# Router scores of the second mixture out of the first mixture's weights: one kernel, before and after

## The chip, the cores and the metric

The kernel runs on one core of a Trainium2 chip. The metric is device time in microseconds of one execution; lower is better. Its engines are TensorE (PE in the profile, its weight loads PEld), VectorE (DVE), ScalarE (ACT), GpSimd (POOL) and SyncE (SP), each with its own queue of instructions; they wait for each other by semaphores only.

## The reference

```python
x = attn(x, weight)            # 4 x 3584 tokens of D = 192; per head softmax(weight) over 7 taps, causal convolution
# first mixture: x is passed through where x @ w_skip <= 0
xc = x[x @ w_skip > 0]
e = argmax(xc @ w_gate); g = softmax(xc @ w_gate)[e]
out = xc + g * (relu(xc @ w1[e]) @ w2[e])         # w1: 192 x 1024, w2: 1024 x 192, 8 experts
# second mixture, all 14336 tokens
e = argmax(x @ w_gate2); g = softmax(x @ w_gate2)[e]
o = sigmoid(x @ w_output_gate2)[e]
out = g * o * (relu(x @ w1_2[e]) @ w2_2[e])
```
Everything is float32. The input of the second mixture's router is the output of the first mixture.

## The kernel before

**Routing.** The tokens are taken in 16 groups (B = 4 batches, GPB = 4) of 7 windows of 128 tokens. For a group SyncE loads the windows (load_windows), TensorE convolves them with Toeplitz matrices (conv, L963, and the halo, L971), ScalarE copies the result into `rows` (rows_out, L527), TensorE transposes the rows (L1026, L1027), ScalarE copies them to x1A and x1B (L545, L546), and TensorE multiplies by routerA and routerB, which hold w_skip, the first mixture's gates and the second's two sets of gates (L1037). The scores are transposed (scores_of, L1006), VectorE chooses the expert, TensorE counts ranks (ranks_of, L993, L995), VectorE works out a slot for each token, and GpSimd scatters each window's rows, with gate and token number behind the 192 values, to a bucket in HBM: seven indirect DMAs a group (L440). Scores, ranks and slots of a group are made in the pass of the next group. `rows` has a buffer for each q of 0 to 3, so rows of group n wait for the scatter of group n-4. A token that skips the first mixture goes straight to a bucket of the second.

**Tiles.** Buckets are read back in tiles of T = 256 tokens, expert by expert, with m = 0 for the first mixture and m = 1 for the second. Every float32 operand is split in a high float32r part and a low rest, so TensorE multiplies three or four terms. In a tile TensorE makes the hidden values (L1095, L1104; 8 and 32 matmuls, into banks 0 to 3), ScalarE the high part of relu (hh, L615), VectorE the low part (hl, h_low, L821), and TensorE the output: 16 products of hh with w2's two parts (L1119, 384 columns) and 16 of hl with its high part (L1126, 192 columns), two for each of FC = 8 slices j and each half of the tile, into banks 4 and 6. VectorE makes the result (result(g)): y_part (L891), y_rows (L897). In between it turns the next tile's blocks (x_turn, L808), splits them (x_low, L814, with x_high on ScalarE, L567) and takes a quarter of the next expert's weights (pieces, L692).

In the first mixture the rows of tile g-1 are routed again during tile g: TensorE transposes y_rows (transpose_y, L1054, L1055), ScalarE copies (yT_copy), TensorE multiplies by the second mixture's gates (scores, L1065, L1066), VectorE chooses (flags, choose, from L837), ScalarE takes exp (L578), VectorE makes the gate (gate, L857 to L863), TensorE the ranks (ranks, L1072, L1074, after slice j = 5), VectorE the slots (places, up to L878). GpSimd copies y_rows to s_rows (L455, `copied`), takes a quarter of w2's low part (L427), and scatters s_rows (L461). The order on each engine is the order of the code; nothing reorders it.

The order in VectorE's loop and on TensorE is what the change and the prediction are about:

```python
h_low(g, 0)
flags(step, g)                  # m == 0 only
for c in range(1, PAIRS): h_low(g, c)        # pieces.one() at c == 2
x_turn(g + 1)
choose(step, g)                 # m == 0 only
x_low(g + 1)
gate(step, g); places(step, g)  # m == 0 only
result(g)
```

## Time and profile before

| | |
|---|---|
| median of 3 runs | 1118.01 us (1116.08 to 1118.71) |
| the profiled execution | 1117.96 us, span 1116.2 us, mean granted TensorE clock 0.976 |
| TensorE busy | 1048.8 us, 94% |
| VectorE, ScalarE, GpSimd busy | 704.9, 528.4, 381.1 us (63, 47, 34%) |
| chain that ended last | TensorE 83%, issue 7%, GpSimd 5%, VectorE 2% |
| DMA | 110.90 MB, 101 GB/s over the span |

Times of instructions come from the one profiled execution, whose own time stands beside its span, so that a sum over its stretches can be held against it. TensorE's matmuls overlap, so the distance from start to start says what one costs, not its duration. The routing takes the first sixth of the span, then follow 33 tiles of the first mixture and 60 of the second. In the routing slices TensorE is 6 to 8 tenths busy, in the tiles 9 or more.

### The profile page before, as it was taken

How to read it: one execution, taken by the hardware profiler on the slowest of the kernel's cores; microseconds unless marked ns; L12 is line 12 of the kernel's file. 1: busy time of each engine (PE TensorE's matmuls, PEld its weight loads, DVE VectorE, ACT ScalarE, POOL GpSimd, SP SyncE). 2: the span in 40 equal slices, each digit the busy share in tenths (PEclk: the TensorE clock that was granted, in tenths of full speed). 3: DMA queues.
4: the chain of work that ended last, by engine and by line, in shares of the span. 5: the costliest groups of instructions: out<-in, count | busy, mean ns of one | idle time of the engine just before them, and what ended most of it. 6: DMA issues, size and time to landing. Idle time of an engine off the chain costs nothing.

```text
span 1116.2 us, 32024 instructions
## 1 busy us (share of the span) xinstructions
PE 1048.8 (94%) x8478; PEld 988.4 (89%) x8479; DVE 704.9 (63%) x2258; ACT 528.4 (47%) x1190; POOL 381.1 (34%) x420
## 2 busy tenths in 40 slices
PE   7887747999999999999699999999999999999997
PEld 6666636999999999999599999999999999999997
DVE  1556654887878888888655555565656555565554
ACT  3445532444545454544245454554545455455443
POOL 2677773232323333333222232222323223223212
PEclk9999977999999999999899999999999999999999
DMA  7855334443433344344253343433434343323222
GB/s 209 241 184 156 101 121 117 98 101 71 96 75 93 89 97 98 82 95 110 71 131 81 75 114 65 113 81 79 113 79 111 64 101 93 65 58 73 61 60 49
DMA packets 252866, 110.90 MB, mean 99 GB/s; under 512 B 170515, under 2 KB 247814, under 8 KB 252848
## 3 DMA queue, kind: packets, MB, share of 16 engines
q1 hardware_dynamic: 210344, 62.19, 26.7%
q0 software_dynamic: 14560, 27.96, 7.1%
q10 hardware_dynamic: 27944, 20.57, 6.8%
q14 instruction: 13, 0.11, 0.0%
q8 instruction: 5, 0.08, 0.0%
HBM read 79.48 MB, written 33.08 MB: 101 GB/s over the span
## 4 chain that ended last, share of the span: by engine, by line
PE 83%; issue 7%; POOL 5%; DVE 2%; ACT 1%; DMA 1%; ACTq 1%; POOLq 0%; SPq 0%; DVEq 0%
PE bank L1104 32%; PE bank L1119 26%; PE bank L1126 12%; PE bank L1095 5%; POOL buckets L440 5%; PE bank L1066 2%; PE bank L1065 1%; PE bank L1054 1%; PE bank L1055 1%; PE bank L963 1%; PE bank L982 1%; DMA buckets<-rows,slot_i 0%; PE bank L1026 0%; ACT rows L527 0%; PE bank L1027 0%
## 5 line engine op out<-in xcount | busy, mean ns | idle before, releaser
L1119 PE MATMUL bank<-w,hh 128*128 128x384 f32 x1488 | 444.4, 361 | 0.4 <-DVE hl L821 0.4
L1126 PE MATMUL bank<-w,hl 128*128 128x192 f32 x1488 | 363.9, 255 | 0.0
L821 DVE SCALAR_TENSOR_TENSOR hl<-bank,hh 128x512 fp32r<-128x512 f32 x372 | 252.8, 690 | 126.7 <-ACT hh L615 123.9
L615 ACT ACTIVATE hh<-bank 128x512 fp32r<-128x512 f32 x372 | 221.6, 599 | 161.0 <-PE bank L1104 147.4
L1126 PEld LDWEIGHTS bank<-w,hl 128*128 128x128 f32 x1488 | 282.9, 191 | 0.0
L1119 PEld LDWEIGHTS bank<-w,hh 128*128 128x128 f32 x1488 | 280.4, 188 | 1.5 <-DVE hl L821 0.6
L466 POOL DMA_INDIRECT out<-y_rows,out_i x120 | 117.3, 978 | 413.4 <-DVE out_i L899 382.1
L1104 PE MATMUL bank<-xAh,w1h 128*128 128x256 f32 x744 | 222.5, 299 | 0.0
L1104 PE MATMUL bank<-xAh,w1l 128*128 128x256 f32 x744 | 210.2, 283 | 0.0
L1104 PE MATMUL bank<-xB,w1h 128*128 128x256 f32 x744 | 208.8, 281 | 0.0
L1104 PE MATMUL bank<-xAl,w1h 128*128 128x256 f32 x744 | 208.4, 280 | 0.0
L1104 PEld LDWEIGHTS bank<-xAh,w1h 128*128 128x128 f32 x744 | 142.0, 191 | 12.8 <-issue 0.7
L1104 PEld LDWEIGHTS bank<-xAh,w1l 128*128 128x128 f32 x744 | 142.0, 191 | 0.0
L1104 PEld LDWEIGHTS bank<-xAl,w1h 128*128 128x128 f32 x744 | 141.5, 190 | 0.0
L1104 PEld LDWEIGHTS bank<-xB,w1h 128*128 128x128 f32 x744 | 141.1, 190 | 0.0
L440 POOL DMA_INDIRECT buckets<-rows,slot_i x112 | 110.5, 987 | 57.2 <-issue 33.5
L461 POOL DMA_INDIRECT buckets<-s_rows,slot_i x68 | 66.9, 984 | 175.6 <-DVE slot_i L878 152.3
L567 ACT CAST xAh<-xT 128x256 fp32r<-128x256 f32 x95 | 38.6, 407 | 162.1 <-DVE xT L809 162.1
L897 DVE SCALAR_TENSOR_TENSOR y_rows<-bank,xkeep,y_part 128x192 f32<-128x192 f32 x186 | 68.6, 411 | 33.2 <-ACT y_part L586 33.2
L814 DVE TENSOR_TENSOR xAl<-xT,xAh 128x256 fp32r<-128x256 f32 x95 | 40.5, 426 | 75.0 <-ACT xC L569 75.0
L586 ACT ACTIVATE y_part<-bank,xkeep 128x192 f32<-128x192 f32 x120 | 44.0, 417 | 88.3 <-PE bank L1119 88.3
L1095 PE MATMUL bank<-xB,w1l 64*128 64x256 f32 x372 | 69.7, 308 | 14.2 <-DVE xB L815 14.2
(157 smaller groups left out, 1367.2 us busy)
## 6 DMA issues: line engine op xcount, KB each, us to landing
xblocks<-buckets SPq DMA_DIRECT2D x570, 32.0 KB, 1.8
xkeep<-buckets ACTq DMA_DIRECT2D x93, 196.0 KB, 2.7
xwin<-x SPq DMA_DIRECT2D x17, 672.0 KB
raw<-w_all SPq DMA_DIRECT2D x56, 192.0 KB
raw<-w_all SPq DMA_DIRECT2D x56, 128.0 KB
raw<-w_all SPq DMA_DIRECT2D x112, 64.0 KB
out<-y_rows,out_i POOLq DMA_INDIRECT x120
buckets<-rows,slot_i POOLq DMA_INDIRECT x112
```

Source lines behind the costliest of these rows:

```text
L440: nc.gpsimd.indirect_dma_start(out=buckets, out_offset=bass.IndirectOffsetOnAxis(ap=slot_i[0:W, q % 2, t:t + 1], axis=0), in_=rows[0:W, q, ...
L461: nc.gpsimd.indirect_dma_start(out=buckets, out_offset=bass.IndirectOffsetOnAxis(ap=slot_i[:, 0, h:h + 1], axis=0), in_=s_rows[:, h, :], i ...
L466: nc.gpsimd.indirect_dma_start(out=out, out_offset=bass.IndirectOffsetOnAxis(ap=out_i[:, h:h + 1], axis=0), in_=y_rows[:, h, 0:D], in_offs ...
L586: nc.scalar.mul(y_part[:, h, :], bank[Y[h]][:, 0:D], xkeep[:, h, GATE:GATE + 1]).then_inc(s["y_part"], 1)
L615: nc.scalar.activation(hh[:, 2 * c:2 * c + 2, :].rearrange("p c t -> p (c t)"), bank[c][:], ACT.Relu).then_inc(s["h_high"], 1)
L814: nc.vector.tensor_tensor(xAl[:], xT[:, 0, :], xAh[:].bitcast(F32), ALU.subtract)
L821: nc.vector.scalar_tensor_tensor(hl[:, 2 * c:2 * c + 2, :].rearrange("p c t -> p (c t)"), bank[c][:], 0.0, h, ALU.max, ALU.subtract).then_ ...
L897: nc.vector.scalar_tensor_tensor(y_rows[:, h, 0:D], bank[Y[h]][:, D:2 * D], gated, y_part[:, h, :], ALU.mult, ALU.add)
L1095: nc.tensor.matmul(bank[c + rows_at][:, u * T:(u + 1) * T], w1l[k0, par, 1, at * 128:(at + 1) * 128], (xB, xC)[rows_at][k0, :], start=(u = ...
L1104: last = nc.tensor.matmul(o, w[:, par, half_, f], xs[:], start=False, stop=(i == 3), skip_group_check=True)
L1119: return nc.tensor.matmul(bank[Y[h]][:, 0:2 * D], hh[:, j, t], w2[:, par, j, :, :].rearrange("p a d -> p (a d)"), start=(j == 0), stop=(j ...
L1126: last = nc.tensor.matmul(bank[Y[h]][:, 0:D], hl[:, j, t], w2[:, par, j, 0, :], start=False, stop=False)
```

## The change

Scores are linear, so the second router's scores of out = x + g * y are x @ G + g * (h @ (w2 @ G)), with G the 16 columns of w_gate2 and w_output_gate2. The change uses this:

- A row in the buckets gets 16 more values, x @ G, which routing has anyway (D = 192, DS = 208, ROW = 212, before 196).
- w2 @ G is made once for each of the first mixture's 8 experts during routing, half an expert in each of the 16 group passes: SyncE loads the half (load_w2_half), TensorE transposes it between ranks_of and the halo, ScalarE copies it (w2tA, w2tB), eight more score matmuls run on it, and VectorE puts the result in `fold`. The window buffers go from four to two.
- w2 in SBUF gets these 16 columns, so the first mixture's output products have 416 and 208 columns. transpose_y, yT_copy and scores go.
- VectorE adds the row's own 16 values (score2). It chooses for tile g-1 at the head of tile g, behind the turning of tile g+1's blocks and ahead of every `hl` of tile g; gate and places stand ahead of the last `hl`, and TensorE's ranks after slice j = 1.
- y_part is ScalarE's in both mixtures. s_rows is y_rows + xkeep, summed by GpSimd, and the load of xkeep waits for it (`copied`).

VectorE in a tile of the first mixture, before: hl is the low part of relu, xT the turned blocks, top to score the choice, y_rows the result.

```order
L821 SCALAR_TENSOR_TENSOR hl<-bank,hh 128x512
...
L827 TENSOR_SCALAR flag<-y_rows 128x2
...
L821 SCALAR_TENSOR_TENSOR hl<-bank,hh 128x512
...
L821 SCALAR_TENSOR_TENSOR hl<-bank,hh 128x512
...
L692 TENSOR_TENSOR w1l<-raw,w1h 128x2x256
...
L808 STREAM_TRANSPOSE xT<-xblocks 128x256
...
L837 TENSOR_REDUCE top<-bank 128x2
...
L851 TENSOR_REDUCE score<-picked 128x2
...
L814 TENSOR_TENSOR xAl<-xT,xAh 128x256
...
L878 TENSOR_TENSOR slot_i<-slot,flag 128x2
...
L891 SCALAR_TENSOR_TENSOR y_part<-bank,xkeep 128x192 x2
```

and of the change:

```order
L855 STREAM_TRANSPOSE xT<-xblocks 128x256
...
L885 TENSOR_REDUCE top<-score 128x2
...
L899 TENSOR_REDUCE score<-picked 128x2
...
L868 SCALAR_TENSOR_TENSOR hl<-bank,hh 128x512
...
L905 TENSOR_REDUCE total<-escore 128x2
...
L926 TENSOR_TENSOR slot_i<-slot,flag 128x2
...
L868 SCALAR_TENSOR_TENSOR hl<-bank,hh 128x512
...
L861 TENSOR_TENSOR xAl<-xT,xAh 128x256
...
L732 TENSOR_TENSOR w1l<-raw,w1h 128x2x256
...
L875 TENSOR_SCALAR flag<-xkeep 128x2
...
L939 SCALAR_TENSOR_TENSOR y_rows<-bank,xkeep,y_part 128x208
...
L944 TENSOR_TENSOR score<-y_rows,xkeep 128x32
```

The turning and the choice moved from behind the four `hl` to ahead of the first, the slots from the end to ahead of the fourth, and the weights' quarter and the flags from the middle to the end.

TensorE in a routing pass, before, from the last ranks matmuls to the scores: x1A and x1B are the transposed rows.

```order
L993 MATMUL bank<-hot_pad,before 128x128
L995 MATMUL bank<-hot_pad,ones 128x128 x7
L963 MATMUL bank<-xwin,toep 128x168 x4
L971 MATMUL bank<-xhalo,toep_halo 32x168 x8
...
L1037 MATMUL bank<-x1A,routerA 32x256 x3
L1037 MATMUL bank<-x1A,routerA 32x128
```

and of the change, w_rawA and w_rawB being the half of w2 as loaded:

```order
L1006 MATMUL bank<-xwin,toep 128x168 x4
L1039 MATMUL bank<-hot_pad,before 128x128
L1041 MATMUL bank<-hot_pad,ones 128x128 x7
...
L1083 MATMUL bank<-ident,w_rawA 128x128 x4
L1085 MATMUL bank<-ident,w_rawB 128x128 x2
L1016 MATMUL bank<-xhalo,toep_halo 32x168 x8
L1095 MATMUL bank<-x1A,routerA 32x256 x3
...
L1105 MATMUL bank<-w2tA,routerA 32x128 x4
L1108 MATMUL bank<-w2tB,routerB 32x128
```

The second half of the convolution moved ahead of the ranks, and the transposes of w2 stand between the ranks and the halo, whose end lets ScalarE write the next rows.

The diff, cut to its core, with eight columns of indentation taken off where there are that many:

```diff
-    ROW = D + 4
-    GATE, TOK = D, D + 1
+    DS = D + 2 * E
+    ROW = DS + 4
+    GATE, TOK = DS, DS + 1
...
-w2 = sb("w2", [128, 2, FC, 2, D], F32R)
+w2 = sb("w2", [128, 2, FC, 2, DS], F32R)
+fold = sb("fold", [128, E + 1, FC, 2 * E])
...
+    def load_w2_half(n, expert):
+
+        two = w2_all[bass.ds(expert, 1), :, :].rearrange("a (c p) d -> p (a c) d", p=128)
+        c = slice(n % 2 * HC, n % 2 * HC + HC)
+        sp.dma_start(w2_rawA[:, n % 2, :, :], two[:, c, 0:128]).then_inc(w2raw_in[n % 2], 16)
+        sp.dma_start(w2_rawB[:, n % 2, :, :], two[:, c, 128:D]).then_inc(w2raw_in[n % 2], 16)
+
+    load_windows(0, 1)
+    for n in range(2):
+        load_w2_half(n, 0)
+    for q in range(2, GPB):
+        sp.wait_ge(conv_ready, q - 1)
         load_windows(0, q)
...
-            sp.wait_ge(conv_ready, b * GPB + q - (GPB - 1))
+            sp.wait_ge(conv_ready, b * GPB + q - 1)
             load_windows(b, q)
-    sp.wait_ge(conv_ready, (B - 1) * GPB + 1)
+            sp.wait_ge(tr_ready, (b * GPB + q) * 3 - 3 * (GPB - 1))
+            load_w2_half(q, b * 2 + (q // 2 - 1))
...
-                nc.gpsimd.tensor_copy(s_rows[:], y_rows[:]).then_inc(s["copied"], 1)
+                nc.gpsimd.tensor_tensor(s_rows[:, :, 0:DS], y_rows[:, :, 0:DS], xkeep[:, :, 0:DS], ALU.add)
+                nc.gpsimd.tensor_copy(s_rows[:, :, TOK], xkeep[:, :, TOK]).then_inc(s["copied"], 1)
...
-        nc.scalar.copy(w2[:, par, d, 0, :], raw2[:, par, d, :]).then_inc(w_high, 1)
+        if m == 0:
+            nc.scalar.copy(w2[:, par, d, 0, D:DS], folded(k, d))
+        nc.scalar.copy(w2[:, par, d, 0, 0:D], raw2[:, par, d, :]).then_inc(w_high, 1)
...
+            act.wait_ge(tr_ready, n * 3 + 3)
+            nc.scalar.copy(w2tA[:], bank[4][:])
+            nc.scalar.copy(w2tB[:], bank[5][:, 0:2 * W]).then_inc(tr_copied, 1)
...
+                            if m == 1:
+                                act.wait_ge(s["yrows_ready"], g + 1)
+                                act.dma_start(xkeep[:], tile_rows(g, off)
+                                              ).then_inc(s["keep_in"], 16)
+                        if c == 2 and m == 0:
+                            exp(g)
+                            act.wait_ge(s["copied"], g + 1)
                             act.dma_start(xkeep[:], tile_rows(g, off)
                                           ).then_inc(s["keep_in"], 16)
-                            if m == 0:
-                                yT_copy(g)
                     x_high(g + 1)
-                    if m == 0:
-                        exp(g)
-                    if m == 1:
-                        y_half(g)
+                    y_half(g)
                     if m == 1:
                         pieces.one()
...
+            nc.vector.tensor_copy(rows[0:W, q, :, D:DS], LG[:, :, 1 + E:NR])
...
+            dve.wait_ge(w2_scored, n + 1)
+            nc.vector.tensor_copy(fold[:, bass.ds(b * 2 + q // 2, 1), q % 2 * HC:q % 2 * HC + HC, :]
+                                  .rearrange("p a c s -> p (a c) s"),
+                                  GW[:, :, 1 + E:NR]).then_inc(fold_ready, 1)
...
-            dve.wait_ge(s["scores"], r + 1)
+            dve.wait_ge(s["yrows_ready"], r + 1)
...
-                dve.wait_ge(s["yT_ready"], g + 1)
             else:
                 dve.wait_ge(s["sent"], g * 32 + 16)
-            for h in range(SUB):
-                gated = xkeep[:, h, GATE:GATE + 1]
-                if m == 0:
-                    nc.vector.scalar_tensor_tensor(y_part[:, h, :], bank[Y[h]][:, 0:D], gated,
-                                                   xkeep[:, h, 0:D], ALU.mult, ALU.add
-                                                   ).then_inc(s["y_part"], 1)
+                nc.vector.tensor_copy(out_i[:], xkeep[:, :, TOK])
             for h in range(SUB):
                 gated = xkeep[:, h, GATE:GATE + 1]
                 dve.wait_ge(s["y_part"], g * SUB + (h + 1))
-                nc.vector.scalar_tensor_tensor(y_rows[:, h, 0:D], bank[Y[h]][:, D:2 * D], gated,
-                                               y_part[:, h, :], ALU.mult, ALU.add)
-            nc.vector.tensor_copy(y_rows[:, :, TOK] if m == 0 else out_i[:],
-                                  xkeep[:, :, TOK]).then_inc(s["yrows_ready"], 1)
-
+                last = nc.vector.scalar_tensor_tensor(y_rows[:, h, 0:width], bank[Y[h]][:, DS:DS + width],
+                                                      gated, y_part[:, h, 0:width], ALU.mult, ALU.add)
+            if m == 0:
+                last.then_inc(s["y_sum"], 1)
+                dve.wait_ge(s["y_sum"], g + 1)
+                last = nc.vector.tensor_tensor(score2[:], y_rows[:, :, D:DS], xkeep[:, :, D:DS], ALU.add)
+            last.then_inc(s["yrows_ready"], 1)
...
                     step = Steps(s["step"], g * STEPS2)
-                    h_low(g, 0)
-                    if m == 0:
-                        flags(step, g)
-                    for c in range(1, PAIRS):
-                        h_low(g, c)
-                        if c == 2 and m == 0:
-                            pieces.one()
                     x_turn(g + 1)
                     if m == 0:
                         choose(step, g)
-                    x_low(g + 1)
+                    for c in range(3):
+                        h_low(g, c)
                     if m == 0:
                         gate(step, g)
                         places(step, g)
+                    h_low(g, 3)
+                    x_low(g + 1)
+                    pieces.one()
+                    if m == 0:
+                        flags(step, g)
                         assert step.n == STEPS2
-                    else:
-                        pieces.one()
                     result(g)
...
+            last_group(q, b, ranks_of)
+            pe.wait_ge(tr_copied, n * 3 + 3)
+            pe.wait_ge(w2raw_in[q % 2], b * 64 + (q // 2 * 32 + 32))
+            for i in range(HC):
+                nc.tensor.transpose(bank[4][:, i * W:(i + 1) * W], w2_rawA[:, q % 2, i, :], ident[:])
+            for i in range(2):
+                last = nc.tensor.transpose(bank[5][:, i * W:(i + 1) * W],
+                                           w2_rawB[:, q % 2, 2 * i:2 * i + 2, :].rearrange("p c d -> p (c d)"),
+                                           ident[:])
+            last.then_inc(tr_ready, 1)
+            halo(n + 1, (q + 1) % GPB)
             pe.wait_ge(scoreT_copied, n + 1)
-            pe.wait_ge(setup_done, 7)
-            for w, xT in ((routerA, x1A), (routerB, x1B)):
-                for k in range(4):
-                    used = 1 if k == 3 else 2
-                    last = nc.tensor.matmul(SC[k * QUAD:(k + 1) * QUAD, 0:used, :], w[:],
-                                            xT[:, 0:used, k * W:(k + 1) * W],
-                                            start=(w is routerA), stop=(w is routerB), skip_group_check=True)
+            pe.wait_ge(setup_done, 8)
+            pe.wait_ge(fold_ready, n)
...
+            pe.wait_ge(tr_copied, n * 3 + 4)
+            for k in range(4):
+                nc.tensor.matmul(SCW[k * QUAD:(k + 1) * QUAD, :], routerA[:], w2tA[:, k * W:(k + 1) * W],
+                                 start=False, stop=False, skip_group_check=True)
+            for k in range(4):
+                last = nc.tensor.matmul(SCW[k * QUAD:(k + 1) * QUAD, :], (routerB, routerC)[k % 2][:],
+                                        w2tB[:, k // 2 * W:(k // 2 + 1) * W], start=False, stop=True,
+                                        skip_group_check=True)
...
-                        if m == 0 and c == 1:
-                            transpose_y(g)
-                    if m == 0:
-                        scores(g)
...
-                                    bank[Y[h]][:, 0:2 * D], hh[:, j, t],
-                                    w2[:, par, j, :, :].rearrange("p a d -> p (a d)"),
+                                    bank[Y[h]][:, 0:2 * DS].rearrange("p (a d) -> p a d", d=DS)[:, :, 0:width],
+                                    hh[:, j, t], w2[:, par, j, :, 0:width],
                                     start=(j == 0), stop=(j == FC - 1))
 
                             if j == 0:
                                 high_terms()
-                            last = nc.tensor.matmul(bank[Y[h]][:, 0:D], hl[:, j, t], w2[:, par, j, 0, :],
-                                                    start=False, stop=False)
+                            last = nc.tensor.matmul(bank[Y[h]][:, 0:width], hl[:, j, t],
+                                                    w2[:, par, j, 0, 0:width], start=False, stop=False)
                             if j > 0:
                                 last = high_terms()
-                        if m == 0 and j == 5:
+                        if m == 0 and j == 1:
```

## Rows read from the trace of the kernel before

**Rows 1.** Page, costliest groups: GpSimd's scatters. Columns: busy, mean ns | idle before, releaser
```profile
L440 POOL DMA_INDIRECT buckets<-rows,slot_i x112 | 110.5, 987 | 57.2 <-issue 33.5
```

**Rows 2.** Waits, 0 to 215 us. Columns: total us, times, longest us
```profile
POOL buckets L440 <- DVE slot_i L763: 23.7, 2, 23.4
```

**Rows 3.** Timeline of TensorE, 80 to 101 us. Columns: start, us, what, [idle before]
```profile
88.21 0.32 PE L1026 MATMUL bank<-ident,rows 128*128 128x128 f32 x1 [1.87 <-ACT rows L527]
...
90.50 0.28 PE L1026 MATMUL bank<-ident,rows 128*128 128x128 f32 x1
90.61 0.27 PE L1027 MATMUL bank<-ident,rows 128*64 128x128 f32 x1
...
94.55 0.80 PE L1037 MATMUL bank<-x1B,routerB 128*32 128x128 f32 x8
97.33 0.47 PE L1026 MATMUL bank<-ident,rows 128*128 128x128 f32 x1 [1.98 <-ACT rows L527]
```

**Rows 4.** Timeline of ScalarE, 80 to 101 us
```profile
95.73 1.47 ACT L527 COPY rows<-bank 128x336 f32<-128x336 f32 x4 [3.33 <-DMA buckets<-rows,slot_i]
```

**Rows 5.** Chain that ended last, 150 to 205 us. Columns: start, us, what
```profile
174.54 2.62 DMA buckets<-rows,slot_i
...
184.04 0.20 PE bank L1072
...
184.66 0.37 PE bank L1119
...
185.19 0.37 PE bank L1119
...
199.64 2.09 PE bank L1104 x16
```

**Rows 6.** Chain that ended last, 530 to 580 us
```profile
532.68 2.07 PE bank L1104 x16
...
550.95 0.16 DVE slot_i L878
...
568.63 3.94 PE bank L1104 x32
...
577.82 2.19 PE bank L1104 x17
```

**Rows 7.** TensorE in a tile of mixture 1, its ranks
```profile
408.47 0.19 PE L1072 MATMUL bank<-hot_pad,before 128*128 128x24 bf16 x1
```

**Rows 8.** Timeline of VectorE in a tile of mixture 1, and at mixture 2's start
```profile
399.55 0.73 DVE L897 SCALAR_TENSOR_TENSOR y_rows<-bank,xkeep,y_part 128x192 f32<-128x192 f32 x2
...
405.60 0.43 DVE L808 STREAM_TRANSPOSE xT<-xblocks 128x256 f32<-128x256 f32 x1
...
406.28 0.12 DVE L837 TENSOR_REDUCE top<-bank 128x2 f32<-128x16 f32 x1
...
407.59 0.43 DVE L814 TENSOR_TENSOR xAl<-xT,xAh 128x256 fp32r<-128x256 f32 x1
...
409.81 0.16 DVE L878 TENSOR_TENSOR slot_i<-slot,flag 128x2 int32<-128x2 f32 x1
...
562.36 2.48 DVE L821 SCALAR_TENSOR_TENSOR hl<-bank,hh 128x512 fp32r<-128x512 f32 x4 [7.16 <-ACT hh L615]
```

**Rows 9.** Timeline: w1l on VectorE, w2's subtraction on GpSimd, w1l again
```profile
404.25 0.82 DVE L692 TENSOR_TENSOR w1l<-raw,w1h  x1
...
404.61 1.34 POOL L427 TENSOR_TENSOR w<-raw,w  x1
...
569.49 0.69 DVE L692 TENSOR_TENSOR w1l<-raw,w1h  x1 [1.91 <-ACT w1h L502]
```

**Rows 10.** Line 247 on VectorE's queue, 206 to 216 us: min/median/max ns, first and last start
```profile
L247 DVEq FUSED_REGOPS  x2: 77/134/190, 211.8 to 212.3; - x2
...
L247 DVEq SEQ_ASSERT  x1: 23/23/23, 212.9 to 212.9; - x1
```

**Rows 11.** Stretch: length, busy of PE, PEld, DVE, ACT, POOL, clock, DMA share, GB/s
```profile
189.00:190.00 1.00, 1.00 (x9) 1.00 (x9) 0.00 (x0) 0.28 (x1) 0.00 (x0) 0.79 0.15 23
```

More of the change, by code:

```diff
@@ L100, in program @@
         scoreT = sb("scoreT", [128, 2, W])
+        w2_rawA = sb("w2_rawA", [128, 2, FC // 2, 128])
+        w2_rawB = sb("w2_rawB", [128, 2, FC // 2, DB])
+        w2tA = sb("w2tA", [128, FC // 2 * W])
+        w2tB = sb("w2tB", [128, 2 * W])
+        scoreW = sb("scoreW", [128, W])
         tok_int = sb("tok_int", [128, GPB * WPG], I32)
@@ L162, in program @@
         scattered = [sem(f"scattered{q}") for q in range(GPB)]
[L163 removed]
+        win_in = [sem(f"win_in{q}") for q in range(2)]
         win_zero, conv_ready, rows_ready, tr_ready, tr_copied = map(sem, (
@@ L556, in _ @@
                         used = HALVES[half] * QUAD
-                        last = nc.scalar.copy(scoreT[0:used, half, :], SC[0:used, half, :])
-                    last.then_inc(scoreT_copied, 1)
-                    last_batches(act, b, lambda k: high(k, k, q))
+                        nc.scalar.copy(scoreT[0:used, half, :], SC[0:used, half, :])
+                    nc.scalar.copy(scoreW[:], SCW[:]).then_inc(scoreT_copied, 1)
+                    last_batches(act, b, lambda k: high(k, 0, k, q))
             exp_of(GPB * B - 1)
@@ L585, in y_half @@
                     for h in range(SUB):
-                        nc.scalar.mul(y_part[:, h, :], bank[Y[h]][:, 0:D],
+                        nc.scalar.mul(y_part[:, h, 0:width], bank[Y[h]][:, 0:width],
                                       xkeep[:, h, GATE:GATE + 1]).then_inc(s["y_part"], 1)
+                width = DS if m == 0 else D
                 x_high(0)
@@ L945, in _ @@
                     step = Steps(s["step"], n * STEPS2)
-                    for part in (flags, choose, gate, places):
+                    for part in (choose, gate, places):
                         part(step, n)
@@ L1008, in scores_of @@
                 last.then_inc(scores_ready, 1)
+                nc.tensor.transpose(bank[7][:, 3 * W:4 * W], scoreW[:], ident[:]).then_inc(w2_scored, 1)
             def last_group(q, b, part):
```

156 lines of the change are left out of this document (80 added, 76 removed).

## The prediction

> **What bounds the kernel now.** I read the chain of waits first, because it splits the span into stretches with different limits, then TensorE's timeline inside one turn of each stretch, then who waits there.
>
> The routing stretch (31 to 175 us) belongs to GpSimd. Its 112 scatters of 987 ns start 1.285 us apart (987 plus 0.30 of issue) and wait for slots only before the first one (23.7 us in two waits, the longest 23.4) [rows 1, 2]. A group of seven costs 8.99 us. TensorE's pass over a group takes 9.12 us (88.21 to 97.33), and of that it idles 1.98 us for `rows` [rows 3]; ScalarE writes those rows after 3.33 us of waiting for an older scatter to land [rows 4]. So TensorE's passes follow GpSimd, with some 2 us of room.
>
> The tiles belong to TensorE. Those of the first mixture turn every 11.10 us ((532.68 - 199.64) / 30), those of the second every 9.19 us [rows 5, 6], and no wait stands inside a tile. Between 198.9 and 543.1 lie tiles 2 to 32 of the first mixture: 31 tiles, out of 33.
>
> **What it removes from a tile.** The two loops differ by 1.91 us, and by TensorE work only: four transposes of y_rows, four score matmuls, and the ranks. The ranks stay; they start at 408.47 between two products [rows 7], and I give them 0.17 us (bounds 0.1 and 0.2, one to three short matmuls). So 1.74 us go.
>
> **What it adds to a tile.** 16 products grow by 32 columns and 16 by 16: 768 columns. 32 products of 256 columns took 3.94 us, 0.48 ns a column [rows 6], so +0.37 us (bounds 0.3, if only the stream counts, and 0.5). The new period is 9.19 + 0.17 + 0.37 = 9.73 us if nobody else is late; 31 tiles x 1.37 = 42.5 us saved.
>
> **Who could be late.** Let T be the start of a tile on TensorE. VectorE now has before its first `hl` all of the head: y_rows (0.73 in [rows 8], some 0.05 more for 16 columns; it needs ScalarE's y_part, which moves there from VectorE and comes at about T+0.6), the score sum (bounds 0.1 and 0.3 by its other small operations, I take 0.2), the turning of x (405.60 to 406.28, 0.68) and the choice (406.28 to 407.59, 1.31). That makes T+3.6, and `hl` of pair 0 is written at T+4.3. TensorE needs it when its first products end, at T+0.67+3.74 = T+4.4. It fits with 0.1 us to spare. The other pieces follow: three `hl` 0.62 apart (four in 2.48) to T+5.5, gate and places 1.5 (from x_low's end, 407.59 + 0.89, to 409.97) to T+7.0, last `hl` to T+7.7 where it is needed at T+8.4, x_low 0.9 to T+8.5, a quarter of w1l 0.75 and the flags 0.37 to T+9.7. The sum of VectorE's work is about 9.0 us in 9.73. Near the limit, but under it.
>
> GpSimd's copy of y_rows becomes a sum with xkeep. No row has this sum; the nearest is its subtraction of 384 columns, 1.34 us [rows 9], so 1.45 us, bounds 0.5 (the copy) and 2. It starts when the last scatters have landed, about T+2.9, since slots are now written at T+7.0 and not at T+11; `copied` comes at T+4.5. Behind it now wait ScalarE's load of xkeep and, in its queue, the relu of pair 3, which is ready at T+4.4 and done at T+5.5: early enough. ScalarE gains two y_part (0.41 each) and a 32-column cast before its first relu, which ends at T+3.1; its room in a normal tile was 0.4 us and pair 0 is now wanted by VectorE at T+3.6 only.
>
> A change of expert is where the cover is gone: VectorE reads the tables for 1.1 us (211.8 to 212.9) [rows 10], before while it waited anyway, now between y_rows and the head. `hl` 0 slips to T+5.1 and TensorE waits 0.7 us: 7 x 0.7 = 4.9 us. For the 24 other tiles I put 0.1 us each for waits that I have as zero, 2.4 us. Net of the tiles: -35.2 us (bounds: -44 without a stall, -15 with 0.9 us per tile).
>
> The Trainium skill (SBUF — State Buffer, section "SBUF: two separate sides") speaks against this placement: VectorE with two SBUF inputs and a reading GpSimd operation hold one port pair exclusively, and the later one is blocked entirely. If GpSimd's 1.45 us sum always fell on the choice or on `xAl`, a tile would pay up to that and the saving would nearly vanish. The rows beside it speak for less: GpSimd's subtraction started at 404.61 within VectorE's w1l operation, and that took 0.82 us where it takes 0.69 with GpSimd idle [rows 9]: 0.13 us, which is about the slip that my sum has.
>
> **Routing.** TensorE gets per pass six transposes at 0.11 us [rows 3], one of scoreW, and eight 32-row products of 128 columns (the last eight instructions of the scores take 0.80 us [rows 3]): about 1.6 us. ScalarE gets three copies of 512, 256 and 128 columns (for 512 columns I estimate 0.5 us, since four copies of 336 take 1.47 [rows 4]), two of them now before the rows. Halo and rows come some 0.9 us later in a pass, while the ranks' wait is covered by the convolution that moves ahead of it. Without the 1.98 a pass is 7.1 us of TensorE's queue, half a microsecond of it a wait for the ranks' input that is now covered; with 1.6 more I get 8.2 (7.8 to 8.7), under 8.99. What remains is one shift: pass 1 starts 0.9 us later, scoreW's transpose and the extra row copy add 0.3, so the first scatter goes at 32.4 and not 31.2. To this 1.1 us for stretches at the low clock, where a pass costs twice. +2.3 us (bounds 0 and 12). On SP's queue a half of w2 (384 KB) now follows each window of 672 KB, after a wait on TensorE's halo; I place its arrival 6.5 us behind that halo and its use at 6.5 to 7. With windows in two buffers and not four it has no further cover but the 1.4 us that the passes wait for GpSimd anyhow.
>
> The skill (DMA: Bandwidth & Descriptors, "Specifications") puts line rate at 512 B or more a piece; w2_rawB is loaded in 256 B pieces, which by it costs a read-modify-write. That would lengthen the smaller third of each half and lean towards rival B; no row here shows such a load alone.
>
> **Hand-over to the tiles.** Before, tile 0 did most of its second products while the last scatters ran, and stopped only at the ranks, which needed the choice behind the turning of x for tile 1. That x came after the last scatter had landed (174.54 + 2.62), and z at 184.0 [rows 5]. Now the turning stands at the head of tile 0, so all its second products wait. The choice ends at about 184.0 again, `hl` 0 at 184.65; then 16 pairs of products. TensorE had been idle and restarted at 184.04 at a granted clock of 0.50 (1.2 GHz); between 189 and 190 the mean is 0.79, so the rise to 2.4 GHz came some 5.3 us after the restart [rows 5, 11]. A pair costs 0.53 there (184.66 to 185.19), with the added columns 0.57: nine in 5.3 us, seven at 0.31 after it. Tile 1 starts at 192.1 and tile 2 at 201.8 and not at 198.97: +2.9 us (bounds 1 and 5).
>
> **From mixture 1 to 2.** Tile 32 ends at 543.1 and the last slots came at 550.95 [rows 6], behind transposes, a copy and scores. Without them: y_rows and sum to +1.6, tables, choice and exp to +3.9, gate and places to +5.4: 2.4 us earlier. But the turning of x for tile 1 now stands before `hl` 0 again, and its data lands about 1.7 us after that was first wanted. -0.7 us (bounds -3 and +1). The second mixture's products keep their width: 0.
>
> **Sum.** -35.2 + 2.3 + 2.9 - 0.7 = -30.7 us. The profiled execution took 1117.96 us (span 1116.2), the median of the runs is 1118.01, so nothing is to be corrected: 1087 us.
>
> **Rivals.**
> A: VectorE becomes the bound of the tile. For it: 9.0 us of work in 9.73, in one strict order, with six waits on others in it. Against it: it has no two waits in a row that I find late. At 10.4 us a tile the saving is 31 x 0.7 = 22 us, and with the other terms 1101 us. Chance 0.15.
> B, the other side: routing leaves GpSimd's pace, because halves of w2 land late behind the windows and TensorE's queue, with halo and all later rows behind it, stands. Beyond 8.99 us each 0.1 us of a pass costs 1.6 us. It decides from 8.99 + 33/16 = 11.1 us; at 12.0 the kernel takes 1087 + 48 = 1135 us. For it: queue order and 256 B pieces, and the low clock doubles TensorE's 8 us. Against it: 1.98 us of idle in each pass and slots one group ahead. Chance 0.08, and 0.03 that it just cancels the gain.
> C: no stall at all and no loss in routing: 1118 - 42.5 - 0.7 + 1.2 + 2.9 = 1079 us, or less if the ranks cost nothing. It is the low end of the forecast, not apart from it.
> D: the change does not do what it says, in that ranks and choice keep TensorE waiting as before: then z at T+3.6 must be missed by over 2 us. I see nothing for it; it is in A.
>
> **How the numbers follow.** Forecast 0.74 (its own range 1077 to 1097), A 0.15, B 0.11 with its middle. The range to hold 8 of 10 reaches from C's lower edge, 1074, to beyond A, 1106. What a measurement of this kernel can tell from no change is about 0.2%, 2.2 us. Faster: forecast and A, less a little of A's tail, 0.87. Same 0.03, slower 0.10.
>
> **What would show it.** In the profile of the changed kernel: first-mixture tiles 9.7 to 9.9 us apart; TensorE waiting for `hl` only at changes of expert, under 1 us; second-mixture tiles still 9.19; GpSimd's scatters still 1.285 us apart with waits for slots under a few us after the first; the first at about 32.4; a hole before tile 0's second products that ends near 187 (184.65 plus the shift of routing). Waits for `hl` in every tile mean A; TensorE waiting for w2_raw or scatters waiting for slots mean B. A period above 10.4 us, or routing more than 12 us longer, makes the prediction wrong.

## The result and the profile after

| | before | after |
|---|---|---|
| median of the runs, us | 1117.25 (1116.08 to 1118.71, 4 runs) | 1144.22 (1140.38 to 1152.85, 4 runs) |
| ratio | 1 | 1.0246, 95% interval 1.0214 to 1.0279 |
| profiled execution, us (span) | 1117.96 (1116.2) | 1145.99 (1144.2) |
| predicted | | 1087 (1074 to 1106) |

The change makes the kernel 2.5% slower, and the prediction missed it by 57 us. The page of the changed kernel, its costliest groups in the form of [rows 1]:

```profile
span 1144.2 us, 32401 instructions
...
PE 1043.0 (91%) x8438; PEld 976.3 (85%) x8439; DVE 727.2 (64%) x2230; ACT 535.7 (47%) x1272; POOL 407.9 (36%) x488
...
PEclk8799996899999999999979999999999999999999
...
PE 67%; DVE 10%; issue 9%; SPq 5%; DMA 3%; POOL 3%; ACT 2%; DVEq 1%; POOLq 0%; ACTq 0%
...
L1167 PE MATMUL bank<-w,hh 128*128 128x384 f32 (+1 forms) x1488 | 458.6, 368 | 48.7 <-DVE hl L868 48.7
...
L478 POOL DMA_INDIRECT buckets<-rows,slot_i x112 | 111.2, 993 | 69.9 <-DVE slot_i L810 37.2
```

and the line of the second products on the page of the kernel before:

```profile
L1119 PE MATMUL bank<-w,hh 128*128 128x384 f32 x1488 | 444.4, 361 | 0.4 <-DVE hl L821 0.4
```

TensorE is busy for 1043 us in a longer span. In front of L1167, the second products of a tile, it idles 48.7 us for VectorE's `hl`, where it was 0.4, and the scatters of the routing stretch (L478) now wait 37.2 us for slots where it was 23.7 [rows 2].

To place the loss I took the first product of each tile on TensorE. The changed kernel's tile 2 of mixture 1, its last tile of mixture 1 and tile 1 of mixture 2:

```profile
218.48 0.38 PE L1147 MATMUL bank<-xB,w1l 64*128 64x256 f32 x1
```
```profile
553.89 0.38 PE L1147 MATMUL bank<-xB,w1l 64*128 64x256 f32 x1
```
```profile
591.25 0.38 PE L1147 MATMUL bank<-xB,w1l 64*128 64x256 f32 x1
```

| stretch | before, us | after, us | difference | predicted |
|---|---|---|---|---|
| start to landing of the last scatter | 177.2 | 192.5 | +15.3 | +2.3 |
| to tile 2 of mixture 1 | 21.8 | 26.0 | +4.2 | +2.9 |
| tiles of mixture 1, from tile 2 to the last | 30 x 11.10 | 30 x 11.18 | +2.4 | -35.2 |
| to tile 1 of mixture 2 | 35.9 | 37.4 | +1.4 | -0.7 |
| the rest, mixture 2 | 59 x 9.19 | 59 x 9.27 | +4.7 | 0 |

The last column sums to -30.7, the one before it to +28. The tiles account for 37.6 us of the miss, routing for 13.

**Inside a tile.** VectorE, GpSimd and TensorE in a tile that begins at T = 409.87; columns are start, duration, instruction, idle time before it and what ended that:

```profile
410.51 0.77 DVE L939 SCALAR_TENSOR_TENSOR y_rows<-bank,xkeep,y_part 128x208 f32<-128x208 f32 x2 [0.78 <-ACT y_part L624]
411.32 0.19 DVE L944 TENSOR_TENSOR score<-y_rows,xkeep 128x32 f32<-128x32 f32 x1
411.96 0.45 DVE L855 STREAM_TRANSPOSE xT<-xblocks 128x256 f32<-128x256 f32 x1 [0.45 <-issue]
...
412.65 0.12 DVE L885 TENSOR_REDUCE top<-score 128x2 f32<-128x16 f32 x1
...
413.43 1.11 DVE L894 TENSOR_TENSOR hot_pad<-order,order_top 128x16 bf16<-128x16 f32 x1
414.57 0.17 DVE L897 TENSOR_TENSOR picked<-hot_pad,score 128x16 f32<-128x16 bf16 x1
...
414.89 1.89 DVE L868 SCALAR_TENSOR_TENSOR hl<-bank,hh 128x512 fp32r<-128x512 f32 x3
```
```profile
413.42 1.08 POOL L493 TENSOR_TENSOR s_rows<-y_rows,xkeep 128x416 f32<-128x416 f32 x1 [3.01 <-DMA buckets<-s_rows,slot_i]
...
414.82 1.00 POOL L465 TENSOR_TENSOR w<-raw,w  x1
```
```profile
415.64 0.46 PE L1167 MATMUL bank<-w,hh 128*128 128x416 f32 x1 [1.04 <-DVE hl L868]
```

The instructions are those that I had summed, and y_rows, score sum and turning have the lengths that I gave them. Two things are new. VectorE issues nothing for 0.45 us before it turns x. And L894, a product of 16 columns into hot_pad that took 0.175 us before the change, takes 1.11: until 0.04 us after GpSimd's sum (413.42 to 414.50) is over. So the first `hl` starts at T+5.0, where I had it start at T+3.6 and written at T+4.3, and TensorE waits 1.04 us. In most tiles it isn't the sum that does this but what follows it, GpSimd's subtraction for w2, which the kernel always had; here in a tile at a change of expert, where the idle time ahead of L855 is 2.06 us:

```profile
388.98 0.45 DVE L855 STREAM_TRANSPOSE xT<-xblocks 128x256 f32<-128x256 f32 x1 [2.06 <-issue]
...
390.54 0.75 DVE L894 TENSOR_TENSOR hot_pad<-order,order_top 128x16 bf16<-128x16 f32 x1
```
```profile
390.26 1.00 POOL L465 TENSOR_TENSOR w<-raw,w  x1
```

Between 240 and 560 us, 27 of 29 executions of L894 overlap such a GpSimd operation, and each ends 0.03 to 0.04 us after that one does; it is the subtraction in 24 and the sum in 3 (mean of the 29: 0.75 us). The sum holds up L887, the second step of the choice, as well, in 19 tiles. TensorE's waits between 240 and 600 us (us in total, times, longest):

```profile
PE bank L1167 <- DVE hl L868: 36.0, 30, 2.4
```

**In routing.** SyncE's queue from 28 us on in the changed kernel (first fence), TensorE's wait that follows from it, and SyncE's queue of the kernel before:

```profile
28.09 1.68 SPq L252 DMA_DIRECT2D raw<-w_all  x3
...
32.32 0.59 SPq L254 DMA_DIRECT2D raw<-w_all  x1
33.30 2.39 SPq L314 DMA_DIRECT2D xwin<-x  x1
35.89 5.57 SPq L318 DMA_DIRECT2D xhalo<-x  x4
...
42.34 0.40 SPq L335 DMA_DIRECT2D w_rawB<-w_all  x1
```
```profile
47.42 1.11 PE L1083 MATMUL bank<-ident,w_rawA 128*128 128x128 f32 x4 [8.44 <-DMA w_rawB<-w_all]
```
```profile
17.68 1.68 SPq L233 DMA_DIRECT2D raw<-w_all  x3
...
22.39 1.24 SPq L235 DMA_DIRECT2D raw<-w_all  x1
23.99 3.33 SPq L295 DMA_DIRECT2D xwin<-x  x1
```

The weights of experts 0 and 1 (3.6 MB, `raw<-w_all`) stand between window 3 and window 4. Before, with four window buffers, they were issued at 17.7 us and windows were ahead of their use. With two buffers they go at 28.1, issue of window 4's halo takes 5.6 us behind them, and w_rawB, the later part of w2's third half, is issued at 42.3 and lands 5.03 us later. TensorE stands for 8.4 us and goes on at the low clock (0.50 from 47 to 53 us); the pass takes 20.1 us where its neighbours take 7.85. Over the whole stretch TensorE waits 16.1 us in 9 for w_rawB, so the other eight waits are 1 us each.

**At the hand-over.** The last scatter and the granted clock (length of the stretch, busy us of PE, PEld, DVE, ACT, POOL, clock, DMA share, GB/s), to be held against [rows 5, 11]:

```profile
189.17 3.33 DMA buckets<-rows,slot_i
```
```profile
196.00:202.00 6.00, 1.86 (x7) 1.82 (x8) 4.19 (x17) 1.82 (x5) 0.00 (x0) 0.50 0.50 125
```

TensorE is busy for 1.86 of these 6 us, at 1.2 GHz: tile 0's second products wait for a choice that stands behind the turning of tile 1's x, as predicted. From landing to tile 1 it is 15.5 us (14.9 predicted, 9.4 before).

### The profile page after: what moved, and what is told of

The parts are those of the page before. It is cut to its first block, busy times and chain, and to the rows that moved or that the text cites. A ratio compares the mean times of both kernels' runs of the same rounds, so it can differ in the third digit from the quotient of the medians.

```text
span 1144.2 us, 32401 instructions
## 1 busy us (share of the span) xinstructions
PE 1043.0 (91%) x8438; PEld 976.3 (85%) x8439; DVE 727.2 (64%) x2230; ACT 535.7 (47%) x1272; POOL 407.9 (36%) x488
## 4 chain that ended last, share of the span: by engine, by line
PE 67%; DVE 10%; issue 9%; SPq 5%; DMA 3%; POOL 3%; ACT 2%; DVEq 1%; POOLq 0%; ACTq 0%
PE bank L1167 26%; PE bank L1156 21%; PE bank L1174 12%; PE bank L1147 3%; POOL buckets L478 3%; DMA w_rawB<-w_all 2%; DVE hot_pad L894 2%; DVE hl L868 2%; ACT y_part L624 1%; SPq L318 1%; DVE y_rows L939 1%; DVE xT L856 1%; PE bank L1006 1%; SPq L252 1%; SPq L365 1%
## 5 line engine op out<-in xcount | busy, mean ns | idle before, releaser
L1167 PE MATMUL bank<-w,hh 128*128 128x384 f32 (+1 forms) x1488 | 458.6, 368 | 48.7 <-DVE hl L868 48.7
L1174 PE MATMUL bank<-w,hl 128*128 128x192 f32 (+1 forms) x1488 | 370.8, 259 | 0.0
L1167 PEld LDWEIGHTS bank<-w,hh 128*128 128x128 f32 x1488 | 283.7, 191 | 56.6 <-DVE hl L868 55.6
L1174 PEld LDWEIGHTS bank<-w,hl 128*128 128x128 f32 x1488 | 287.1, 194 | 0.1
L868 DVE SCALAR_TENSOR_TENSOR hl<-bank,hh 128x512 fp32r<-128x512 f32 x372 | 241.0, 679 | 27.8 <-ACT hh L654 27.3
L1156 PE MATMUL bank<-xAh,w1h 128*128 128x256 f32 x744 | 219.8, 295 | 0.0
L624 ACT ACTIVATE y_part<-bank,xkeep 128x192 f32<-128x192 f32 (+1 forms) x186 | 68.9, 422 | 311.7 <-PE bank L1167 311.7
L478 POOL DMA_INDIRECT buckets<-rows,slot_i x112 | 111.2, 993 | 69.9 <-DVE slot_i L810 37.2
L732 DVE TENSOR_TENSOR w1l<-raw,w1h (+1 forms) x64 | 44.3, 692 | 89.7 <-ACT w1h L541 88.4
L939 DVE SCALAR_TENSOR_TENSOR y_rows<-bank,xkeep,y_part 128x192 f32<-128x192 f32 (+1 forms) x186 | 69.8, 416 | 38.2 <-ACT y_part L624 38.2
L855 DVE STREAM_TRANSPOSE xT<-xblocks 128x256 f32<-128x256 f32 x95 | 42.0, 443 | 55.7 <-issue 30.9
```

The costliest lines, as they stand in the source:

```text
L478: nc.gpsimd.indirect_dma_start(out=buckets, out_offset=bass.IndirectOffsetOnAxis(ap=slot_i[0:W, q % 2, t:t + 1], axis=0), in_=rows[0:W, q, ...
L624: nc.scalar.mul(y_part[:, h, 0:width], bank[Y[h]][:, 0:width], xkeep[:, h, GATE:GATE + 1]).then_inc(s["y_part"], 1)
L732: nc.vector.tensor_tensor(w1l[:, par, :, c], raw1[:, par, :, c], w1h[:, par, :, c].bitcast(F32), ALU.subtract).then_inc(w_low1, 1)
L868: nc.vector.scalar_tensor_tensor(hl[:, 2 * c:2 * c + 2, :].rearrange("p c t -> p (c t)"), bank[c][:], 0.0, h, ALU.max, ALU.subtract).then_ ...
L939: last = nc.vector.scalar_tensor_tensor(y_rows[:, h, 0:width], bank[Y[h]][:, DS:DS + width], gated, y_part[:, h, 0:width], ALU.mult, ALU.add)
L1156: last = nc.tensor.matmul(o, w[:, par, half_, f], xs[:], start=False, stop=(i == 3), skip_group_check=True)
```

## Experiments

Nine kernels. The ratio of each is to the kernel before on the same chip, and is to be compared with the 1.0246 of the change.

**1. Each half of w2 loaded one pass earlier.**

```
+            sp.wait_ge(tr_ready, 3)
+            load_w2_half(2, 1)
...
-                    sp.wait_ge(tr_ready, (b * GPB + q) * 3 - 3 * (GPB - 1))
-                    load_w2_half(q, b * 2 + (q // 2 - 1))
+                    sp.wait_ge(tr_ready, (b * GPB + q) * 3 - 6)
+                    load_w2_half(q + 1, b * 2 + ((q + 1) // 2 - 1))
...
```


> Each half of w2 is loaded one group pass earlier than in the changed kernel (as soon as its buffer is free). Theory 1: routing is longer because TensorE stands for these loads; then the waits of the w2 transposes for the DMA go, scatters keep 1.285 us apart from the start, the last one lands near 178 us and not at 192, and the time falls by 11 to 14 us to about 1131. Rival 1: the added work of TensorE and ScalarE makes the pass long, the late load is only what ends last; then the wait moves to rows or copies and the time falls by under 4 us, to 1140 or more. Both: the tiles are unchanged, 11.16 us in the mean.

Measured: 1143.86 us, ratio 1.0217 (1.0178 to 1.0256). The ordinary passes fall to 7.85 us, so their 1 us for w_rawB was real, but the long pass stays at 18.6, the last scatter starts only 3.9 us earlier, and the tiles give it back (11.40 apart in this execution). The expected 11 to 14 us didn't come. TensorE now waits 8.1 us at once for window 4's halo, which stands behind the same weights. The lateness of w2 is not the main loss in routing.

**2. GpSimd starts its sum after VectorE's choice.** Its subtraction for w2, next in its program, moves with it.

```
                         settle(pool)
+                        pool.wait_ge(s["z"], r + 1)
                         nc.gpsimd.tensor_tensor(s_rows[:, :, 0:DS], y_rows[:, :, 0:DS], xkeep[:, :, 0:DS], ALU.add)
```


> GpSimd waits for the end of VectorE's choice before it sums y_rows and xkeep. Theory 2: VectorE's small operations with two SBUF inputs are blocked whole by GpSimd's 1.08 us sum (hot_pad 0.72 us in the mean against 0.175 before); then hot_pad is back at 0.18, the first hl comes 0.8 us earlier, a tile takes 10.3 us in the mean and the time falls by about 25 us to 1119. Rival 2: VectorE's order alone makes it late, or the later copied holds xkeep's load and the last relu back by as much; then the tile stays above 10.9 us and the time within 5 us of 1144.

Measured: 1116.26 us, ratio 0.9972 (0.9949 to 0.9996): 28 us back with one wait. TensorE's waits for `hl` in the same stretch, and L895, the same product into hot_pad (busy us, mean ns):

```profile
PE bank L1168 <- DVE hl L869: 10.3, 7, 3.3
```
```profile
L895 DVE TENSOR_TENSOR hot_pad<-order,order_top 128x16 bf16<-128x16 f32 x30 | 5.2, 175 | 1.0
```

The product is back at 175 ns, and from the choice's start to the first `hl` it is the 1.31 us of the prediction in an ordinary tile. Tiles are 10.29 us apart on average (11.18 in the changed kernel), the ordinary ones mostly 9.87 to 10.04.

**3. x turned behind the third `hl`, in both mixtures.**

```
-                            x_turn(g + 1)
                             if m == 0:
                                 choose(step, g)
                             for c in range(3):
                                 h_low(g, c)
+                            x_turn(g + 1)
```


> The turning of the next tile's blocks stands behind the third hl and not at the head, in both mixtures. Theory 3: the head is too long, 0.7 us of it is the turning, and in the tile 0 of each mixture it holds back all hl; then a tile takes about 10.5 us in the mean (0.65 less), tile 1 starts 4 us earlier against the last scatter, and the time falls by 22 to 26 us to about 1120. If the port is the only cause (theory 2), GpSimd's sum catches the choice elsewhere and still blocks it: then only some 10 us are won, half of them at the two hand-overs.

Measured: 1114.56 us, ratio 0.9947 (0.9917 to 0.9978).

```profile
PE bank L1167 <- DVE hl L868: 14.7, 11, 2.2
```
```profile
L894 DVE TENSOR_TENSOR hot_pad<-order,order_top 128x16 bf16<-128x16 f32 x29 | 10.8, 371 | 1.0
```

GpSimd still holds VectorE up (371 ns, not 175), but with 0.8 us taken from the head (y_rows to choice takes 1.33 us in an ordinary tile and not 2.14) it no longer reaches TensorE in most ordinary tiles: 9.61 to 9.65. At a change of expert it does, mostly 12 to 13.6. Tiles are 10.50 apart on average. Some 0.3 us of VectorE's idle time now stand ahead of the choice, so not all of the 0.45 belongs to the turning. Landing to tile 1 falls from 15.5 to 10.2 us, so the hand-over's cost was the turning.

**4. The three together.**

> The three edits together. If theories 1 to 3 are each right and separate, tiles are bound by TensorE: 9.8 to 9.9 us, routing as in e1, and the time is 1085 to 1092, faster than the kernel before by 2.5%. If the rivals hold, the gains do not add up and it stays above 1110.

Measured: 1092.55 us, ratio 0.9756 (0.9732 to 0.9779). Tiles are 9.93 apart on average, 9.64 in the ordinary case and, but for the first, 10.2 to 10.8 at a change of expert. One pass of 17.1 us stays in routing. The time is just above the range of 1085 to 1092.

**5. The weights of experts 0 and 1 in eighths, one behind each w2 half in b = 1 and 2.** For this the loop over b is written out; nothing else is changed.

```
-            load_weights(sp, 0, 0)
-            load_weights(sp, 1, 1)
-            with sp.Fori(1, B) as b:
+            for b in range(1, B):
                 for q in range(GPB):
...
                     load_w2_half(q, b * 2 + (q // 2 - 1))
+                    if b < 3:
+                        load_weights(sp, b - 1, b - 1, slice(q * (F // PIECES), (q + 1) * (F // PIECES)),
+                                     slice(q * (FC // PIECES), (q + 1) * (FC // PIECES)), 16)
```


> The changed kernel with one difference: the 3.6 MB of weights of experts 0 and 1 are no longer issued in one piece between window 3 and window 4, but in eighths, one behind each w2 half of the passes of b = 1 and 2. Theory (one queue in order: window 4 and w2's second half stood behind 3.6 MB, which made one pass 20.1 us against 7.85 of its neighbours): that pass falls to 8-9 us, first to last scatter falls from 154.7 to 143-146 us (before: 143.3), tile 2 of mixture 1 begins at 207-210 instead of 218.5, the tiles stay as they are (11.2 apart), and the time is 1133 to 1137. Rival (the w2 halves asked for late, the 1.6 us more of TensorE's work and the lower clock lose it in every pass, and the long pass only gathered it): the long pass shrinks but others stretch to 9-11, first to last scatter stays above 151, and the time is 1141 to 1145.

Measured: 1133.95 us, ratio 1.0141 (1.0123 to 1.0158). The long pass is 8.9 us, first to last scatter 145.5 us (154.7 in the changed kernel, 143.3 before), tile 2 starts at 206.5, tiles are 11.22 apart. The rival had the time above 1141. What is left of routing's loss here, 2.1 us from first to last scatter, is all that w2's lateness and TensorE's added work cost. Whether it is the place in the queue or the bytes moving at once that held window 4 and w2 up, this run doesn't tell apart: it takes both away.

**6. GpSimd copies y_rows in place of the sum.** The kernel leaves out the adding of x to the rows that are sent on, so mixture 2 works on other values; the rows and slots are the same.

```
-nc.gpsimd.tensor_tensor(s_rows[:, :, 0:DS], y_rows[:, :, 0:DS], xkeep[:, :, 0:DS], ALU.add)
+nc.gpsimd.tensor_copy(s_rows[:, :, 0:DS], y_rows[:, :, 0:DS])
```


> The changed kernel with GpSimd's sum y + x replaced by a plain copy of y_rows into s_rows at the same place (leaves out the adding of x to the rows that are sent on). Theory (what locks VectorE out is GpSimd reading two operands; a copy with one operand leaves VectorE alone): VectorE's product into hot_pad (L894), mean 0.73 us in the changed kernel, falls to about its 0.175 of before, TensorE's waits for hl in 240-600 us fall from 36 to 10-15 us, tiles 9.9-10.3 apart, time 1116 to 1121. Rival (any GpSimd work over SBUF at this place blocks it for as long as it lasts, 0.6-0.9 us for the copy): L894's mean stays at 0.45-0.7, tiles 10.7-11.1 apart, time 1133 to 1142.

Measured: 1140.14 us, ratio 1.0202 (1.0179 to 1.0225); tiles 11.04 apart. My theory falls: operands aren't what counts. The product into hot_pad, then one moment on VectorE and GpSimd:

```profile
L894 DVE TENSOR_TENSOR hot_pad<-order,order_top 128x16 bf16<-128x16 f32 x30 | 16.3, 543 | 1.0
```
```profile
359.98 0.12 DVE L885 TENSOR_REDUCE top<-score 128x2 f32<-128x16 f32 x1
360.13 0.30 DVE L887 TENSOR_TENSOR is_top<-score,top 128x16 f32<-128x16 f32 x1
...
360.67 0.17 DVE L892 TENSOR_REDUCE order_top<-order 128x2 f32<-128x18 f32 x1
360.88 1.00 DVE L894 TENSOR_TENSOR hot_pad<-order,order_top 128x16 bf16<-128x16 f32 x1
```
```profile
359.87 0.53 POOL L493 COPY s_rows<-y_rows 128x416 f32<-128x416 f32 x1 [1.99 <-DMA buckets<-s_rows,slot_i]
...
360.84 1.01 POOL L465 TENSOR_TENSOR w<-raw,w  x1
```

L887 (360.13) is held until the one-operand copy ends at 360.40, and L894 until w2's subtraction ends at 361.85. Between 240 and 560 us five products of the choice end 0.03 us after such a copy, and 18 of L894 after the subtraction. The copy is half as long as the sum (0.53 for 1.08 us), so it mostly ends earlier, and the subtraction behind it, now earlier too, takes its place. The reductions L885 and L892 have the same 0.12 and 0.17 us with and without an overlap, and the transposes too. The rival, held up by any GpSimd work, had the time right (1133 to 1142).

**7. The edits of 4 and 5 together.**

> The three edits together (w2 halves a pass earlier, GpSimd's sum behind VectorE's choice, x_turn behind the third hl) and the weights of experts 0 and 1 in eighths during b = 1 and 2. Theory (the queue order): the 17.1 us pass that was left goes, the last scatter starts at 176-177 instead of 181.8, tiles stay 9.93 apart, and the time is 1085 to 1088 against 1092.6. Rival (GpSimd's pace of scatters had already made up for that pass, or the eighths now delay the windows of b = 1 and 2): last scatter at 180-183, time 1090 to 1094.

Measured: 1087.17 us, ratio 0.9722 (0.9703 to 0.9742), the fastest version here. The last scatter starts at 176.97, tiles are 9.90 apart. That this is the very number of my forecast is partly luck: mixture 2 costs 5.0 us that I had as zero, and the hand-over (-0.2) and the step to mixture 2 (-2.2), both with the turning out of the head, come out lower than forecast. One tile of it on VectorE and GpSimd:

```profile
402.31 0.17 DVE L895 TENSOR_TENSOR hot_pad<-order,order_top 128x16 bf16<-128x16 f32 x1
...
402.84 1.93 DVE L869 SCALAR_TENSOR_TENSOR hl<-bank,hh 128x512 fp32r<-128x512 f32 x3
```
```profile
402.99 1.10 POOL L494 TENSOR_TENSOR s_rows<-y_rows,xkeep 128x416 f32<-128x416 f32 x1 [2.29 <-DVE score L900]
```

GpSimd's sum now lies beside three `hl`, which read PSUM. These take 1.93 us, and the three in the changed kernel, beside the subtraction, 1.89; with GpSimd idle four took 2.48, so three 1.86 [rows 8]. No hold-up there.

**8 and 9. Why is mixture 2 slower?** Its tiles do the same work, yet turn every 9.27 us and not 9.19. One run gives the kernel before the changed kernel's layout of w2 and of the sums in PSUM (rows 208 floats apart, 192 used), the other only shifts the tensors behind w2 to the same addresses.

```
-        w2 = sb("w2", [128, 2, FC, 2, D], F32R)
+        w2 = sb("w2", [128, 2, FC, 2, D + 16], F32R)
...
-                                            bank[Y[h]][:, 0:2 * D], hh[:, j, t],
-                                            w2[:, par, j, :, :].rearrange("p a d -> p (a d)"),
+                                            bank[Y[h]][:, 0:2 * (D + 16)].rearrange("p (a d) -> p a d", d=D + 16)[:, :, 0:D],
+                                            hh[:, j, t], w2[:, par, j, :, 0:D],
```


> The kernel before with w2's rows in SBUF and the sums in PSUM laid out as in the changed kernel: 208 floats apart, of which 192 are used, in place of 192 (same instructions, same numbers). Theory (this layout makes mixture 2 slower: the 128x384 product now reads and writes two runs with a gap): the period of mixture 2 goes from 9.19 to 9.23-9.27 us, 59 tiles, mixture 1 as much per tile, together +3 to +7 us. Rival (something else, such as addresses or the length of the program): period 9.19 and a time within 0.2% of before.

```
         w2 = sb("w2", [128, 2, FC, 2, D], F32R)
+        unused = sb("unused", [128, 2 * FC * 2 * 16])
```


> The kernel before with 512 unused floats a partition behind w2 in SBUF, so that every tensor declared after w2 lies at the address that it has in the run with the gaps, while w2 itself stays packed. Theory (addresses of the operands in SBUF set the pace of the products, since in the run with the gaps the 256-column products, which never read w2, lengthened from 278 to 280 ns): period of mixture 2 9.21 us, time 2 to 5 us above before. Rival (the gaps in w2 and in PSUM did it): period 9.19, time within 0.2% of before.

Measured: with the gap 1123.42 us, ratio 1.0037 (1.0024 to 1.0050), period 9.217, under the 9.23 to 9.27 expected; with the shift alone 1118.85, ratio 0.9998 (0.9985 to 1.0010), period 9.187. TensorE's products from 600 to 1100 us (busy us, mean ns), with the gap and with the shift:

```profile
L1119 PE MATMUL bank<-w,hh 128*128 128x384 f32 x864 | 255.0, 359 | 0.0
...
L1104 PE MATMUL bank<-xAl,w1h 128*128 128x256 f32 x437 | 122.3, 280 | 0.0
```
```profile
L1120 PE MATMUL bank<-w,hh 128*128 128x384 f32 x876 | 257.7, 358 | 0.0
...
L1105 PE MATMUL bank<-xAl,w1h 128*128 128x256 f32 x432 | 119.9, 278 | 0.0
```

The layout costs something and the shift of addresses costs nothing. The products' own durations don't show where: of the four groups of 256 columns two are 1 to 2 ns longer with the gap (278 to 280 in the one shown), the other two 1 to 2 ns shorter. And the layout explains 0.03 us of the 0.08 a tile; the versions of the changed kernel lie between 9.23 and 9.27, with instructions for TensorE that hardly differ, and the rest stays open.

## Why the prediction was wrong, point by point

- **What bounds before:** right. GpSimd paces routing and TensorE the tiles.
- **TensorE's own part of a tile** (9.19 + 0.17 + 0.37 = 9.73 us): right. Ordinary tiles of runs 3, 4 and 7 turn every 9.64.
- **The step that failed: "the choice (406.28 to 407.59, 1.31)" at T+3.6, "0.1 us to spare", and with it 24 x 0.1 + 7 x 0.7 us of stalls.** The durations were read where GpSimd was idle beside them. In the new place GpSimd's sum and subtraction lie on the choice, and it takes up to 1 us more. My own times already put one on the other: the sum from T+2.9 to T+4.35, the choice to T+3.6. And VectorE's idle time ahead of the turning of x, put down to issue, is 0.45 us more (2.06 at a change of expert). Run 2 keeps the order as predicted and takes the overlap away: 10.29 us a tile and not 11.18, so the overlap is 0.89 of the 1.21 us that a tile is above the 9.97 that my sum of 35.2 us makes over 31 tiles. That the other 0.32 are the idle time is argued, not shown; no run takes it away alone. Without the turning in the head it is 10.50 (run 3), with both changes 9.93.
- **The rule that I weighed and set aside** (the Trainium skill, SBUF — State Buffer, "SBUF: two separate sides"): the trace agrees with it, and had done so before. I read VectorE's w1l at 0.82 for 0.69 us as the price of an overlap [rows 9]. But w1l came first there; the later one was GpSimd's subtraction, 1.34 us where it takes 1.00 alone (390.26 above). And w1l's own 0.13 us fit another overlap, in which it was the later one: GpSimd's copy ran from 404.02 to 404.53, and in the six tiles where such a copy started ahead of w1l and was still running, w1l ends 0.55 to 0.57 us after it and takes 0.68 to 0.92. A second place in the kernel before shows it with an earlier overlap, VectorE's w1l and GpSimd's copy, which takes 0.51 us alone:

```profile
248.89 0.68 DVE L692 TENSOR_TENSOR w1l<-raw,w1h  x1
```
```profile
248.91 1.03 POOL L455 COPY s_rows<-y_rows 128x392 f32<-128x392 f32 x1 [2.26 <-DMA buckets<-s_rows,slot_i]
```

  The choice itself was touched in the kernel before, in five tiles. L839 reads the scores from PSUM and keeps its 0.17 us beside the subtraction; L842 reads two tensors in SBUF and takes 0.22 (0.32 at most) where it takes 0.18 alone, until the subtraction is over:

```profile
295.33 0.17 DVE L839 TENSOR_TENSOR is_top<-bank,top 128x16 f32<-128x16 f32 x1
...
295.54 0.22 DVE L842 TENSOR_TENSOR order<-is_top,revv 128x16 f32<-128x16 f32 x1
```
```profile
294.72 1.01 POOL L427 TENSOR_TENSOR w<-raw,w  x1
```

  The change also moved the scores from PSUM into SBUF. So L887, the L839 of before, can now be held too: between 240 and 600 us it takes 0.34 us in the mean where it took 0.175. No run here leaves the scores in PSUM. Waiting on an engine with slack had no price, and so it didn't look like one. What I called the vanishing of the saving is what came.
- **Routing, +2.3 us (bounds 0 and 12):** +15.3. GpSimd's pace had room for w2's lateness (run 1) and for TensorE's added work (run 5), as argued. The term left out was one of order: I listed the w2 halves behind each window, and not that the 3.6 MB of weights, on the same queue, move in time because the windows ahead of them now wait for buffers. Without that 10 us come back. Its mechanism is that of rival B, w2 landing late with TensorE's queue behind it, in one pass and not in all. The ordinary pass, which I had at 8.2 us, takes 7.85 where nothing is late (run 1); ScalarE's copy of 512 columns, which I put at 0.5 us, takes 0.58 in the kernel before, too little to matter. The Trainium skill's rule on pieces under 512 B (DMA: Bandwidth & Descriptors, "Specifications") isn't needed for any of it; no run here loads such pieces alone. The first scatter, predicted at 32.4, starts between 31.2 and 34.5 in runs whose routing up to there is alike, so that term was below what one execution shows.
- **Hand-over, +2.9:** +4.2, mechanism right (run 3). **Mixture 1 to 2, -0.7 (bounds -3 and +1):** +1.4, just outside; with the turning behind the third `hl` the stretch takes 33.2 us (run 3), 2.7 less than before.
- **Mixture 2, 0:** +4.7. I took equal work for equal time; about a third is the gap in w2's rows.
- **Rivals:** A (VectorE the bound, 1101 us) had the right symptom, waits for `hl` in every tile, but I priced it at 10.4 us a tile since I looked for it in VectorE's own sum of work. B had the right sign. That both came, at 11.2 us a tile, was in none of them.

The change's own idea holds: with its two collisions and the queue's order taken away it gives 1087 us, 2.8% under the kernel before.

## What to carry to other kernels

Durations of small VectorE operations hold only for the neighbours that they were measured beside: where a change moves a chain of them into the head of a tile, lay GpSimd's operations over it in time, and read an overlap in the trace from the side of the instruction that started later. When buffers of a queue's first user are halved, follow everything behind it on that queue, once-only loads too. And a head of dependent steps with 0.1 us to spare has none.

## What the runs showed of the hardware

- VectorE's operations between two tensors in SBUF stand still while GpSimd works on SBUF, be it a sum (1.08 us), a subtraction (1.01) or a copy of one operand (0.53), and end 0.03 us after it. Reductions (0.12, 0.17) and transposes (0.45, 0.40) beside the same work keep their times to 0.01 us, and so does `hl`, with one operand in PSUM (in run 7 0.68 in the mean beside that work and 0.69 without). GpSimd's scatters don't hold w1l up: it takes 0.69 beside them. GpSimd in turn is held by VectorE's w1l (1.03 for 0.51).
- Products of 384 columns whose operand and sum lie in two runs of 192 with a gap of 16 lengthen the tile from 9.187 to 9.217 us.
